# In odd steps of an attention kernel, TensorE computes the large scores ahead of the transposes

## The reference

```python
q_pool = q.reshape(B, H, S // factor, factor, D).mean(axis=3)
scores = scale * np.matmul(q_pool, k.transpose(0, 1, 3, 2))
scores = scores - np.max(scores, axis=-1, keepdims=True)
attn = np.exp(scores)
attn = attn / (np.sum(attn, axis=-1, keepdims=True) + 1e-09)
attn_out = np.matmul(attn, v).astype(np.float32)
x = np.ascontiguousarray(attn_out.transpose(0, 2, 1, 3)).reshape(B * S, H * D)
h = x @ w_in
g = np.maximum(h, 0.0) + alpha * np.minimum(h, 0.0)
return (g @ w_out).astype(np.float32)
```

## Time and profile before

| | |
|---|---|
| median of 3 runs | 889.04 us (888.99 to 889.9) |
| the profiled execution | 888.61 us |
| its span | 886.8 us |
| PE busy | 861.6 us (97%) |
| DVE busy | 514.7 us (58%) |
| ACT busy | 422.4 us (48%) |
| POOL busy | 204.8 us (23%) |

### The profile page before, as it was taken

The page is one execution under the profiler, slowest core; times in us unless marked ns, Lnnn a source line. Parts: engine busy times, 40 slices in busy tenths (PEclk is TensorE's granted clock), DMA queues, the critical chain, the costliest instruction groups (busy, mean ns, idle before and its releaser), DMA issues. The chain is left out here.

```text
span 886.8 us, 20078 instructions
## 1 busy us (share of the span) xinstructions
PE 861.6 (97%) x6631; PEld 618.1 (70%) x6631; DVE 514.7 (58%) x792; ACT 422.4 (48%) x935; POOL 204.8 (23%) x170
## 2 busy tenths in 40 slices
PE   8899999999999999999999999999999999999997
PEld 5455555555555555555557999998999998999996
DVE  4677777777777777777674344444434445444443
ACT  3666666666666666666663222225222224222222
POOL 3101111110101111110403322333223323233230
PEclk9999999999999999999999999999999999999999
DMA  8725644464435634464122212123222222321211
GB/s 196 174 58 135 152 94 115 97 152 116 122 95 125 152 94 111 101 152 113 48 86 69 60 59 71 59 60 107 84 70 61 59 66 88 109 59 59 63 43 72
DMA packets 42670, 84.37 MB, mean 95 GB/s; under 512 B 7568, under 2 KB 15760, under 8 KB 42640
## 3 DMA queue, kind: packets, MB, share of 16 engines
q1 hardware_dynamic: 40640, 80.06, 35.2%
q10 hardware_dynamic: 2000, 3.93, 1.3%
HBM read 79.18 MB, written 4.79 MB: 95 GB/s over the span
## 5 line engine op out<-in xcount | busy, mean ns | idle before, releaser
L763 PE MATMUL slot_ps<-ff 128*128 128x384 f32 x1152 | 217.8, 337 | 1.4 <-PEq L760 1.4
L763 PEld LDWEIGHTS slot_ps<-ff 128*128 128x128 f32 x1152 | 204.3, 188 | 11.1 <-issue 3.3
L546 DVE TENSOR_REDUCE neg_max<-s_ps 128x1 f32<-128x1152 f32 x144 | 194.7, 1352 | 18.1 <-DVEq L545 17.4
L779 PE MATMUL s_ps<-ff 128*128 128x512 f32 x720 | 182.3, 394 | 1.7 <-PEq L777 1.3
L677 PE MATMUL s_ps<-k_f,q_f 64*128 64x512 f32 (+1 forms) x640 | 159.2, 620 | 1.3 <-PEq L729 1.1
L443 ACT ACTIVATE e_sb<-s_ps,neg_max 128x1024 f32<-128x1024 f32 x144 | 159.6, 1109 | 0.0
L710 PE MATMUL pv_ps<-pt,v_f 128*64 128x256 f32 (+1 forms) x1152 | 155.1, 412 | 0.2 <-PEq L729 0.2
L779 PEld LDWEIGHTS s_ps<-ff 128*128 128x128 f32 x720 | 133.4, 188 | 26.0 <-issue 3.0
L710 PEld LDWEIGHTS pv_ps<-pt,v_f 128*64 128x64 f32 x1152 | 76.7, 136 | 95.9 <-issue 52.6
L598 DVE TENSOR_SCALAR e_sb<-slot_ps,alpha_sb 128x384 f32<-128x384 f32 x96 | 59.3, 617 | 113.2 <-DVEq L596 113.2
L580 DVE COPY pt<-slot_ps 128x512 f32<-128x512 f32 x144 | 98.6, 685 | 39.1 <-DVEq L579 39.1
(11 more groups left out here) (47 smaller groups left out, 525.6 us busy)
## 6 DMA issues: line engine op xcount, KB each, us to landing
k_f<-in_k SPq DMA_DIRECT2D x64, 288.0 KB, 4.2
q_raw<-in_q SPq DMA_DIRECT2D x62, 288.0 KB, 4.1
wi_raw<-in_w_in SPq DMA_DIRECT2D x48, 256.0 KB, 2.6
wo_raw<-in_w_out SPq DMA_DIRECT2D x48, 256.0 KB, 2.6
v_f<-in_v SPq DMA_DIRECT2D x32, 288.0 KB, 3.7
out<-pt ACTq DMA_DIRECT2D x5, 768.0 KB, 4.1
inv_bc<-sums SPq DMA_DIRECT2D x32, 80.0 KB, 3.7
k_end<-in_k SPq DMA_DIRECT2D x64, 32.0 KB, 3.9
```

The costliest lines, as they stand in the source:

```text
L546: nc.vector.tensor_reduce(out=neg_max[:, b:b + 1], in_=s_ps[:, S_AT[b]:S_AT[b] + NKEY], op=ALU.max, axis=AX_X, negate=True).then_inc(max_r ...
L763: ins = nc.tensor.matmul(slot_ps[h][:, 0:TOK], w[i][:, d * P:(d + 1) * P], x[h][:, d * TOK:(d + 1) * TOK], start=(d == 0 and w is wi_hi an ...
L779: ins = nc.tensor.matmul(y_ps[h][t], g[h][:, t * P:(t + 1) * P], w[i], start=(first == 0 and j == 0), stop=(last == 1 and j == 2))
```

## The change

In TensorE's `step`, the wait for `exp_done`, the waits of `begin_scores` and the large scores are put into a function. Even steps call it where this code stood, behind the transposes. Odd steps call it first, ahead of the waits for free slots and of the transposes. No other engine's program is changed.

```diff
+            def large_scores(s, left):
+                if left >= 0:
+                    pe.wait_ge(exp_done, 1).then_inc(exp_done, -1)
+                if left > 1:
+                    if s % 2 == 0 or s == 1:
+                        begin_scores(s + 2)
+                    for ins in big_scores(s + 2):
+                        ins.then_inc(s_ready, 1)
+
             def step(s, pair, left=2):
                 t, g = s % TILES, s // TILES % 2
+                if s % 2 == 1:
+                    large_scores(s, left)
                 if s > 0:
                     for i in range(2):
                         pe.wait_ge(slot_free[i], 1).then_inc(slot_free[i], -1)
@@ -725,13 +736,8 @@
                                                       ident[rows, rows])
                             if a == 2 * CH - 1:
                                 ins.then_inc(tr_ready[i], 1)
-                if left >= 0:
-                    pe.wait_ge(exp_done, 1).then_inc(exp_done, -1)
-                if left > 1:
-                    if s % 2 == 0 or s == 1:
-                        begin_scores(s + 2)
-                    for ins in big_scores(s + 2):
-                        ins.then_inc(s_ready, 1)
+                if s % 2 == 0:
+                    large_scores(s, left)
                 if s % 2 == 0:
```

## The result

The changed kernel takes 923.15 us (median of 4 runs, 922.24 to 924.69) against 889.1 us (median of 4): a ratio of 1.0385, 95% interval 1.0372 to 1.0398, slower by 34 us. The profiled execution took 922.41 us with a span of 920.6 us.

The account below looks back on a forecast made before the run. TensorE, busy 97% of the span, was taken as the bound. Longer pairs of steps added 4.36 us a period, 34.9 over eight, less about 1 at the end: +34, giving 923.0 us, range 907 to 936.

Parts of the forecast that it names:

- (1): TensorE's own work in odd steps, scores to transposes to product: 1.56 us before, 1.57 after, 0 to 6 us in all.
- (2): TensorE's earlier wait for exp_done: without 0.55 us of transposes as cover, each odd step stalls at least 0.29 us.
- (3): Closed loop over ScalarE, VectorE and TensorE: 6.63 us from one odd step's scores to the next, against 5.15 before.
- (4): Attention-stage pairs of steps longer than the rest: two with a VectorE inversion 6.98 us, two with the longest product 7.15.
- (5): Attention stage: nine pairs 61.41 us a period against 57.05, +34.9 over eight, last two steps about -1: +34 us.
- only the first loss: Rival: only the 0.29 us stall before odd steps' scores counts, no loop; 903 to 910 us, chance 0.09.
- Faster: Rival: VectorE's odd-step reduction follows its scores, starting nearer B+1.1 than B+2.96 (B: scores' start); 870 us, chance 0.04.
- No difference: Rival: TensorE takes the waiting out elsewhere, needing the exponential 0.29 us earlier; 889 us, chance 0.03.
- The clock: Rival: idling brings TensorE's 1.2 GHz level in a tenth of the periods; 968 us, within 0.08 for above 936.

## Why the prediction was right

It gave 923.0 us and 923.15 was measured, in a range of 907 to 936. The steps:

(1) *PE's own work unchanged.* Right. Scores to transposes 0.94 us (262.44 to 263.38; 0.93 predicted), transposes to product 0.62 (0.64). With the waits removed the steps take what they took before. One form was outside: where the scores come as eight matmuls on 64 columns the transposes follow at 1.02 us (235.51 to 236.53), the upper bound named.

(2) *The lost cover.* Right. The exponential's start to the scores is 1.35 us (1.34), the wait stands before every odd step, and alone it costs 14.1 us. The prediction gave 14 to 21 for a kernel that had only this loss.

(3) *The loop.* Right link by link. Behind the scores: copy 1.71 us (1.76 predicted), small exponential 2.21 (2.25), reduction 2.91 (2.96), small exponential of the odd tile 4.39 (4.44), copy 4.75 (4.80), large exponential 5.23 (5.29), next scores 6.58 (6.63). The first link is 0.05 short, because the transposes' block lasts 0.69 instead of 0.71 us and the copy follows 0.08 behind it; the rest was carried on.

(4) *The two longer kinds.* With an inversion 6.94 and 6.93 (6.98). VectorE's timeline of the changed kernel, the copy and the reduction around it, 1.51 us apart (1.49):

```profile
216.34 0.69 DVE L580 COPY pt<-slot_ps 128x512 f32<-128x512 f32 x1 [0.51 <-DVEq L579]
...
217.85 1.36 DVE L546 TENSOR_REDUCE neg_max<-s_ps 128x1 f32<-128x1152 f32 x1
```

With the longest product 7.07 (7.15): I took 4.49 us from one transposes to the next for both, of which the changed kernel shows 4.40 (248.80 to 253.20); the 4.49 had a wait for the exponential in it.

(5) *The sum.* 61.15 us a period against 61.41 predicted, 32.8 against 34.9 us over eight. The ends of the stage were put at -1 and are +1.0 (33.8 less 32.8), so two errors of 2 us cancel. For the -1 the prediction had no row, and the runs show why it was wrong. PE's timeline of these two steps, in the changed kernel:

```profile
497.74 0.71 PE L735 MATMUL slot_ps<-ident,e_sb 64*128 64x64 f32 x16
...
500.80 0.72 PE L735 MATMUL slot_ps<-ident,e_sb 64*128 64x64 f32 x16 [1.90 <-PEq L730]
501.44 2.38 PE L710 MATMUL pv_ps<-pt,v_f 128*64 128x320 f32 x16
```

and in the kernel before:

```profile
464.96 0.71 PE L724 MATMUL slot_ps<-ident,e_sb 64*128 64x64 f32 x16
...
466.70 0.72 PE L724 MATMUL slot_ps<-ident,e_sb 64*128 64x64 f32 x16 [0.52 <-PEq L719]
467.64 2.37 PE L710 MATMUL pv_ps<-pt,v_f 128*64 128x320 f32 x16 [0.22 <-PEq L729]
```

The last odd step has no large scores left, but it keeps the early wait for `exp_done`. The product starts 3.70 us behind the transposes of the step before instead of 2.68, which makes up the +1.0. That the total is within 0.2 us of the median is luck of that size; the pairs, within 0.1 us, are what the method gives. The first pair of the table, put 0.07 too low, has its reduction 0.12 us late in both kernels (3.04 and 2.87 us, where like pairs have 2.91 and 2.74); the cause stays open. The pair at 235.51, put 0.08 too low, begins with the eight matmuls named in (1).

The rivals: *only the first loss* was put at 903 to 910, and the kernel that has only this loss gave 903.23; it isn't the changed kernel, since the delayed transposes, over both copies, add 20 us. *Faster* fell at the point that the prediction named: the reduction starts 2.91 us behind the scores and not near 1.1, and the wait before the ninth blocks (64.1 against 65.4 us) didn't shrink. *No difference* needed an earlier exponential, and the waits before L677 show that it doesn't come earlier. *The clock* stayed at its upper level with a wait of 0.2 to 0.6 us in each odd step of the period shown, 1.00 in its row. The section of the Trainium skill cited there (TensorE: Matmul & The Clock Gate, "A second HAM failure mode: psum-queue depth-cycling") tells of a kernel whose clock swings with frequent short waits; this trace has such waits and doesn't show it.

## What to carry to other kernels

Moving work ahead on the bound engine takes away the cover of whatever it waits for, and delays what it used to feed; count both, and follow each along the other engines' fixed orders until it comes back to where it began. If the sum of links around such a loop exceeds the engine's own work, idle engines don't help: pairs of different work take the same time. Here it became shorter when a link was taken out or put elsewhere in an engine's order. A slow link found so (here the inversion) was worth moving to where the bound engine's work hides it, even though the change that led there is to be dropped.

## What the runs showed that was not expected

In this kernel a wait that comes late had to be the last of a row of waits. Two waits for signals that were already there, queued behind the late one on TensorE, added 0.33 us (1.67 against 1.34) from exponential to transposes, with entries 0.15 and 0.18 us apart, and 17.5 us to the kernel. In the prediction this wasn't a term because the change puts the late wait right ahead of the scores; had the slot waits stood between the two, the stall would, by an estimate from these 0.33 us, have been 0.62 instead of 0.29 us.
